# Retention and two gated MLPs on one core: first tile kept in SBUF, folding quarters and weight splits moved

## What is computed

```python
scores = (1 / sqrt(64)) * (q @ k.T)              # 8 batches x 8 heads, 576 x 576, head size 64
ret    = scores * gamma[h] ** (i - j), 0 for i < j
x      = ret @ v                                 # as 4608 tokens x 512
h      = max(max(x @ w1, x @ w2), x @ w3)        # 512 -> 768
x2     = h @ w_out                               # 768 -> 512
a, b   = x2 @ u1, x2 @ u2                        # 512 -> 1024
out    = ((a * b) @ u3) @ u_out                  # 1024 -> 1024 -> 512
```

## Time and profile before

| | us |
|---|---|
| three runs | 1256.33, 1257.79, 1263.64 |
| their median | 1257.79 |
| the profiled execution | 1263.11 |
| its span, first to last instruction | 1261.3 |
| TensorE busy in it | 1229.0 (97%) |
| VectorE, ScalarE, GpSimd busy | 774.1, 487.2, 434.0 |

### The profile page before, as it was taken

One profiled execution on the slowest core, in us unless ns is written; L12 is line 12 of the kernel. 1 busy time (PEld: TensorE's weight loads), 2 busy tenths in 40 slices (PEclk: granted clock), 3 DMA queues, 4 the chain that ended last, 5 costly groups with the idle time before them and its releaser, 6 DMA issues. The chain is left out here.

```text
span 1261.3 us, 21125 instructions
## 1 busy us (share of the span) xinstructions
PE 1229.0 (97%) x8288; PEld 1211.0 (96%) x8288; DVE 774.1 (61%) x1186; ACT 487.2 (39%) x771; POOL 434.0 (34%) x228
## 2 busy tenths in 40 slices
PE   7899999999999999999999999999999999999999
PEld 7798889999999999999999999999999999999998
DVE  5565676764645454558789767554545465867563
ACT  3333344432323242426455444242424243545441
POOL 2635536502020202033786564202020216266540
PEclk9899999999999999999999999999999999999999
DMA  9899865212020302033545441212121343444441
GB/s 328 313 333 349 297 235 160 86 47 79 26 101 26 100 26 95 32 126 126 192 163 198 163 169 57 102 64 106 50 101 57 107 156 123 151 150 151 156 157 64
DMA packets 87828, 174.15 MB, mean 138 GB/s; under 512 B 9648, under 2 KB 58416, under 8 KB 87728
## 3 DMA queue, kind: packets, MB, share of 16 engines
q1 hardware_dynamic: 79088, 163.94, 37.0%
q10 hardware_dynamic: 8640, 8.85, 2.0%
HBM read 109.32 MB, written 63.44 MB: 137 GB/s over the span
## 5 line engine op out<-in xcount | busy, mean ns | idle before, releaser
L1057 PE MATMUL ps<-chi,whi 128*128 128x384 f32 x2016 | 675.5, 335 | 11.6 <-DVE clo L795 5.9
L1059 PE MATMUL ps<-chi,wlo 128*128 128x384 f32 x2016 | 674.1, 334 | 0.0
L1058 PE MATMUL ps<-clo,whi 128*128 128x384 f32 x2016 | 674.1, 334 | 0.0
L554 POOL TENSOR_TENSOR raw<-raw,raw 128x768 f32<-128x768 f32 (+2 forms) x96 | 267.3, 2804 | 591.5 <-DMA raw<-xd 222.1
L1057 PEld LDWEIGHTS ps<-chi,whi 128*128 128x128 f32 x2016 | 378.9, 188 | 15.8 <-issue 7.9
L1058 PEld LDWEIGHTS ps<-clo,whi 128*128 128x128 f32 x2016 | 378.9, 188 | 0.0
L1059 PEld LDWEIGHTS ps<-chi,wlo 128*128 128x128 f32 x2016 | 378.9, 188 | 0.0
L795 DVE TENSOR_TENSOR clo<-raw,chi 128x768 fp32r<-128x768 f32 (+2 forms) x168 | 251.9, 1527 | 27.7 <-ACT chi L712 27.7
L712 ACT CAST chi<-raw 128x768 fp32r<-128x768 f32 (+2 forms) x168 | 180.3, 1080 | 86.0 <-PE ps L1059 52.3
L785 ACT COPY w<-ps 128x384 f32<-128x384 f32 x126 | 60.7, 482 | 253.4 <-PE ps L1059 252.0
L771 ACT COPY u<-ps 128x384 f32<-128x384 f32 x126 | 60.8, 482 | 161.8 <-PE ps L1059 160.1
(11 more groups left out here) (41 smaller groups left out, 857.0 us busy)
## 6 DMA issues: line engine op xcount, KB each, us to landing
qks<-qk SPq DMA_DIRECT2D x32, 576.0 KB, 7.0
gd<-h SPq DMA_DIRECT2D x96, 192.0 KB, 1.9
raw<-gd SPq DMA_DIRECT2D x24, 768.0 KB, 5.9
hd<-h SPq DMA_DIRECT2D x72, 192.0 KB, 1.9
raw<-hd SPq DMA_DIRECT2D x24, 576.0 KB, 5.6
vs<-vv SPq DMA_DIRECT2D x32, 320.0 KB, 8.4
raw<-xd SPq DMA_DIRECT2D x24, 384.0 KB, 5.7
x2d<-h SPq DMA_DIRECT2D x48, 192.0 KB, 2.1
```

Of the source, the lines that this page charges most:

```text
L554: return nc.gpsimd.tensor_tensor(out_, a, b, op)
L1057: nc.tensor.matmul(to, w1, x1, start=(start and k == 0), stop=False, skip_group_check=True)
L1058: nc.tensor.matmul(to, w1, x2, start=False, stop=False, skip_group_check=True)
L1059: last = nc.tensor.matmul(to, w2, x1, start=False, stop=(k == KH[st] - 1), skip_group_check=True)
```

## The change

- Outputs of the attention that belong to tile 0 (all of the first batch, the first 192 tokens of the second) are copied by ScalarE from PSUM into tile 0's raw blocks, and neither stored nor loaded. Later pairs go through three buffers `xst` in place of two, and SP issues their stores, behind v's loads.
- v is loaded as 512 columns and a tail of 64 rows; the zeros of the tail are set once by six memsets.
- The quarters are spread 0 in steps 0 to 3, 1 in steps 4 to 7, 2 in steps 8 to 11, 4 in steps 12 to 16. `uo` is loaded one piece per step in steps 2 to 5, `u3raw` in steps 1, 6, 8, 10 to 14, now behind the queries' load. GpSimd splits `uo` behind the queries.
- Weight blocks 9, 10, 19 and 20 are split one unit earlier, 20 is loaded one unit earlier, 11 to 13 are split at the end of the unit before (AT_ONCE), and the tokens of tile 0 of O are split at other points.

```diff
-HI_IO = {("prev", "w"): [0], ("end", "u"): [1], ("end", "p3"): [2], ("end", "p2"): [3],
+HI_IO = {("prev", "p3"): [0], ("end", "u"): [1], ("end", "p3"): [2], ("end", "p2"): [3],
...
-LO_IO = {("end", "21"): [0], ("end", "12"): [1], ("next", "22"): [2, 3], ("next", "12"): [4, 5, 6]}
+LO_IO = {("prev", "12"): [0], ("end", "12"): [1], ("next", "22"): [2, 3], ("next", "21"): [4],
+         ("next", "12"): [5, 6]}
...
-             18: 69, 19: 109, 20: 112}
+             18: 69, 19: 109, 20: 111}
...
-W_SPLIT_AT = {wi: it + (wi >= FIRST_W[C]) for wi, it in W_SUM_AT.items()}
+W_SPLIT_AT = {wi: it + (FIRST_W[I] <= wi < FIRST_W[O]) for wi, it in W_SUM_AT.items()}
+
+AT_ONCE = (11, 12, 13)
...
-WC_FROM = 3
-QUARTERS = 4 * FT2
+QUARTERS = [0] * 4 + [1] * 4 + [2] * 4 + [4] * 5
 
 
...
-    if m >= STEPS - 2:
-        return range(QUARTERS - 4 * (STEPS - m), QUARTERS - 4 * (STEPS - m) + 4)
-    return range(2 * (m - WC_FROM), 2 * (m - WC_FROM) + 2) if m >= WC_FROM else ()
...
-U3_LOAD = {min(2 * kb + WC_FROM - 2, STEPS - 3): kb for kb in range(FT2)}
-U3_SPLIT = {min(2 * kb + WC_FROM - 1, STEPS - 2): kb for kb in range(FT2)}
-UO_LOAD = {1: (0, 1), 2: (2, 3)}
-UO_SPLIT = {2: (0, 1), 3: (2, 3)}
-WC_READ = {min(2 * kb + WC_FROM + 1, STEPS - FT2 + kb): kb for kb in range(FT2)}
+    return range(sum(QUARTERS[:m]), sum(QUARTERS[:m + 1]))
+
+
+assert len(QUARTERS) == STEPS and sum(QUARTERS) == 4 * FT2
+
+U3_LOAD = {1: 0, 6: 1, 8: 2, 10: 3, 11: 4, 12: 5, 13: 6, 14: 7}
+U3_SPLIT = {3: 0, 7: 1, 9: 2, 11: 3, 12: 4, 13: 5, 14: 6, 15: 7}
+UO_LOAD = {2: 0, 3: 1, 4: 2, 5: 3}
+UO_SPLIT = {3: 0, 4: 1, 5: 2, 6: 3}
+WC_READ = {7: 0, 9: 1, 11: 2, 12: 3, 13: 4, 14: 5, 15: 6, 16: 7}
 P1_W_LOAD = {8: 0, 9: 1}
 P1_W_SUM = {9: (0, 0), 10: (0, 1), 11: (1, 0), 12: (1, 1)}
 P1_W_HI = {11: 0, 13: 1}
 P1_W_LO = {12: (0, 0), 13: (0, 1), 14: (1, 0), 15: (1, 1)}
-P1_RAW = 9
+
+TILE0 = [[(0, N, {0: 0, 1: 2}, 0), (N, SEQ, {0: 3, 1: 6}, 0)], [(0, 2 * N - SEQ, {0: 3, 1: 6}, SEQ - N)]]
+X_STORES = [0 if n < PAIRS else 1 if n < 2 * PAIRS else 2 for n in range(NP)]
+
+
+def x_stores(n):
+    return sum(X_STORES[i] for i in range(n % 3, n + 1, 3))
+
+
 P1_T = {10: 0, 11: 1, 12: 2, 13: 3}
 P1_HI = {12: 0, 13: 1, 14: 2, 15: 3}
 P1_LO = {13: 0, 14: 1, 15: 2, 16: 3}
 
 
-def build(nc, qk, vv, kk, wB, wC, wI, u3T, uo, decay, qdecay, vdecay, outT):
+def build(nc, qk, vv, vt, kk, wB, wC, wI, u3T, uo, decay, qdecay, vdecay, outT):
     f32, f32r = mybir.dt.float32, mybir.dt.float32r
     ALU = mybir.AluOpType
...
+        xst = at("xst", [P, 3, SEQ], f32, A21_AT + 3 * KH[B] * P * 4)
+        assert A21_AT + 3 * KH[B] * P * 4 + 3 * SEQ * 4 <= H_AT + 4 * N * 4
 
...
-                sp.dma_start(vs[n % 6][:, :], vv[n, :, :]).then_inc(v_loaded[n % 6], 16)
+                sp.dma_start(vs[n % 6][:, 0:NC * CH], vv[n, :, :]).then_inc(v_loaded[n % 6], 16)
+                sp.dma_start(vs[n % 6][TAIL:P, NC * CH:], vt[n, :, :]).then_inc(v_loaded[n % 6], 16)
 
...
                 half = 3 * b // 2
                 cut = N if b % 2 == 0 else SEQ - N
-                for i, (lo, hi) in enumerate(((0, cut), (cut, SEQ))):
-                    to = 0 if (b % 2 == 0 or i == 1) else N - cut
-                    sp.dma_start(acts[B][half + i, p // 2, :, p % 2, to:to + hi - lo], xst[:, n % 2, lo:hi]
-                                 ).then_inc(x_stored[n % 2], 16)
+                pieces = ((0, cut, 0 if b % 2 == 0 else N - cut), (cut, SEQ, 0))
+                for i, (lo, hi, to) in enumerate(pieces):
+                    if i >= 2 - X_STORES[n]:
+                        sp.dma_start(acts[B][half + i, p // 2, :, p % 2, to:to + hi - lo], xst[:, n % 3, lo:hi]
+                                     ).then_inc(x_stored[n % 3], 16)
 
             def load_u3(kb):
...
+                    load_weight(P1_W_LOAD[m])
+                for n in made_in(m + 2):
+                    load_qk(n)
                 if m in U3_LOAD:
                     load_u3(U3_LOAD[m])
-                for i in UO_LOAD.get(m, ()):
-                    load_uo(i)
-                if m in P1_W_LOAD:
-                    load_weight(P1_W_LOAD[m])
-                if m == P1_RAW:
-                    load_raw(0)
-                for n in made_in(m + 2):
-                    load_qk(n)
                 for n in (2 * m, 2 * m + 1):
                     if n + 4 < NP:
                         load_v(n + 4)
+                    if n - 2 >= PAIRS:
+                        store_x(n - 2)
                 if m in WC_READ:
                     store_wc(WC_READ[m])
-            for n in (NP - 2, NP - 1):
-                store_x(n)
 
...
             for m in range(STEPS - 1):
-                if m in U3_SPLIT:
+                if m in U3_SPLIT and m not in UO_SPLIT:
                     split_u3(U3_SPLIT[m])
-                for i in UO_SPLIT.get(m, ()):
-                    split_uo(i)
                 if m in P1_W_SUM:
                     sum_weight(*P1_W_SUM[m])
                 if m in P1_T:
                     combine(0, P1_T[m])
                 for n in made_in(m):
                     decay_queries(n)
+                if m in UO_SPLIT:
+                    if m in U3_SPLIT:
+                        split_u3(U3_SPLIT[m])
+                    split_uo(UO_SPLIT[m])
 
...
-                if n >= 2:
-                    act.wait_ge(x_stored[n % 2], 32 * (n // 2))
-                nc.scalar.copy(xst[:, n % 2, :],
-                               ps[:, 2 * (n % 2):2 * (n % 2) + 2, :].rearrange("p a b -> p (a b)")[:, 0:SEQ]
-                               ).then_inc(x_out, 1)
-
-            def store_x(n):
-                b, p = divmod(n, PAIRS)
-                act.wait_ge(x_out, n + 1)
-                half = 3 * b // 2
-                cut = N if b % 2 == 0 else SEQ - N
-                for i, (lo, hi) in enumerate(((0, cut), (cut, SEQ))):
-                    to = 0 if (b % 2 == 0 or i == 1) else N - cut
-                    act.dma_start(acts[B][half + i, p // 2, :, p % 2, to:to + hi - lo], xst[:, n % 2, lo:hi]
-                                 ).then_inc(x_stored[n % 2], 16)
+                x = ps[:, 2 * (n % 2):2 * (n % 2) + 2, :].rearrange("p a b -> p (a b)")
+                in_tile = TILE0[b] if b < 2 else []
+                for i, (lo, hi, block, to) in enumerate(in_tile):
+                    copy = nc.scalar.copy(raw[B][block[p // 2]][:, p % 2, to:to + hi - lo], x[:, lo:hi])
+                if X_STORES[n]:
+                    if n - 3 >= PAIRS:
+                        act.wait_ge(x_stored[n % 3], 16 * x_stores(n - 3))
+                    lo = in_tile[-1][1] if in_tile else 0
+                    copy = nc.scalar.copy(xst[:, n % 3, lo:SEQ], x[:, lo:SEQ])
+                copy.then_inc(x_out, 1)
 
             def split_uo(i):
...
                         split_weight(wi, 1)
+                for wi in AT_ONCE:
+                    if W_SPLIT_AT[wi] == it:
+                        split_weight(wi, 0)
+                        split_weight(wi, 1)
                 if it < G:
                     act.wait_ge(prod, DONE[(it, P7)])
...
             for i in range(2):
                 nc.vector.memset(state[i][:, :, :], 0.0).then_inc(zeroed, 1)
-            dve.wait_ge(zeroed, 6)
+            for i in range(6):
+                nc.vector.memset(vs[i][0:TAIL, NC * CH:], 0.0).then_inc(zeroed, 1)
+            dve.wait_ge(zeroed, 12)
             for m in range(STEPS):
```

More of the change, by code:

```diff
@@ L309, in build @@
         x_out = sem("x_out")
-        x_stored = [sem(f"x_stored{i}") for i in range(2)]
+        x_stored = [sem(f"x_stored{i}") for i in range(3)]
         uo_loaded = [sem(f"uo_loaded{i}") for i in range(4)]
@@ L431, in load_raw @@
                 if st == B:
-                    for i in range(2):
-                        sp.wait_ge(x_stored[i], 32 * (4 if t == 0 else NP // 2))
+                    for n in range(NP - 3, NP):
+                        sp.wait_ge(x_stored[n % 3], 16 * x_stores(n))
                 else:
@@ L438, in load_raw @@
                 if t == 0:
-                    if st != B:
-                        sp.wait_ge(c_lo, 7 * tau)
+                    sp.wait_ge(c_lo, 7 * tau)
                     if st == C:
@@ L581, in combine @@
                     for k in (0, 1):
-                        pool.wait_ge(raw_loaded[k], 16 * (tau + 1))
+                        pool.wait_ge(raw_loaded[k], 16 * tau)
+                    if tau == 0:
+                        pool.wait_ge(x_out, 2 * PAIRS)
                     if again:
@@ L588, in combine @@
                 if i == 1:
-                    pool.wait_ge(raw_loaded[2], 16 * (tau + 1))
+                    pool.wait_ge(raw_loaded[2], 16 * tau)
                     pool.wait_ge(combined, 4 * tau + 1)
@@ L598, in combine @@
                 if i == 3:
-                    pool.wait_ge(raw_loaded[3], 16 * (tau + 1))
+                    pool.wait_ge(raw_loaded[3], 16 * tau)
                     pool.wait_ge(combined, 4 * tau + 2)
@@ L644, in decay_values @@
```

(27 more changed lines are left out.)

5 lines of the change are left out of this document (4 added, 1 removed).

## The result

| | us |
|---|---|
| before, median of 4 runs | 1258.14 |
| changed, median of 4 runs | 1272.70 (1270.78 to 1275.85) |
| ratio, 95% interval | 1.0111 (1.0073 to 1.0148) |
| span of the profiled execution, before and changed | 1261.3, 1270.4 |
| first product of the later stages at | 193.04, 206.42 |

The change made the kernel 1.1% slower where 1.1% faster was forecast, and the time lies outside the range. The later stages take 4.3 us less. The first stage takes 13.4 us more. Step 8 starts at 81.22 and not at 91.53, so up to there the changed kernel is 10.3 us ahead; it loses 23.7 us behind that point.

What follows compares the result with a forecast made beforehand. Bound: TensorE, nearly always busy in 1068.3 us of later products, and a first stage losing 16.4 us to stalls. Span 1261.3 - 9.1 - 8.0 = 1244.2, plus 1.8 is 1246.0; less half of 5.3, 1243.5 us; range 1234 to 1254.

Steps and rivals of the forecast that it cites:

- What bounds the kernel now: First stage: TensorE's steps should take 153.3 us from step 2 but take 169.7, so 16.4 us are lost.
- First tile kept: First stage: dropping early stores and read back aims at 3.5 + some 2.8 us and slow clock (4.6 + 1.8).
- Quarters moved: First stage: the new spread sums to 155.6 us, 2.3 more than before, paying only through avoided stalls.
- Stalls that stay: Steps 3 to 11: transfers leave 0 to 9 us of stall, 5 taken; stage ends at 183.9, -9.1 us (-14 to -4).
- Stores on SP's queue: First stage: up to 16 issues per step on SP, costed at nothing beyond the 5 us of stall.
- Rival D: First stage: SP's issues become the bound, 13.3 us a step instead of 9.5, +34 us, 1278; chance 0.05.
- Later stages: Behind 193 us: earlier weight splits remove TensorE's waits, -8.0 us (-10.6 to -3), with new waits of 0.6 us three times.
- B: First stage: transfers bound it anyway at 318 GB/s, 9 us of stall stay, stage -0.5, 1252; chance 0.24.
- E: Later stages: the new split place costs as much as the old, -3 there, 1248.5; chance 0.12.
- a slower one: Whole kernel: a time above the 1% bound of 1270.4 us; chance 0.06.

Runs made afterwards that it cites:

- e8: e7 with the stores of the finished pairs issued by ScalarE and not SP; 1243.9 us, 0.9857 of the kernel before.
- e13: e8 with v loaded in one piece of 640 columns again, zeros included; 1244.5 us, 0.9884 of the kernel before.
- e12: e8 with two buffers for the finished pairs in place of three; 1248.4 us, 0.9925 of the kernel before.
- e6: e3 with the stores of the finished pairs issued by ScalarE, quarters spread as in the change; 1248.8 us, 0.9918 of the kernel before.
- e4: The kernel before with only the later stages' edits (weight and token splits moved, block 20 loaded earlier); 1257.5 us, 0.9968 of the kernel before.
- e14: e8 with weight block 9 of stage C split a unit later, where it was before the change; 1242.5 us, 0.9867 of the kernel before.
- e1: The changed kernel with SP issuing u3's load ahead of the step's weights and queries; 1251.5 us, 0.9941 of the kernel before.
- e7: e1 with quarters, uo and u3 loads and splits, and GpSimd's order as in the kernel before; 1250.0 us, 0.9907 of the kernel before.
- e3: The changed kernel with u3 loaded ahead of the queries and its low part behind the queries' decays on GpSimd; 1248.9 us, 0.9923 of the kernel before.
- e5: The changed kernel with the stores of the finished pairs issued by ScalarE, three buffers kept; 1267.7 us, 1.0055 of the kernel before.

## Why the prediction was wrong

**What bounds the kernel now**: right. The losses of the first stage were where it put them; with the tile kept and the ring loosened they go (e8: steps 4 to 12 all at 10.12 or 10.13 us).

**First tile kept**: right. With old quarters and ScalarE's stores the first product comes 12.5 us earlier (193.0 to 180.5). That the tile carries most of it is shown by exclusion only, since no run has the tile alone: with v whole the gain stays (e13), and with two buffers it stays in the trace's first stage (180.9), though the times are some 4 us longer (e12). One cost put at nothing was not nothing: in e8 TensorE waits 1.8 us at step 3 for the copies into the raw blocks, which ScalarE makes behind its rounding of `uo`.

**Quarters moved**: the sum was 2.3 us more for TensorE, and e6 against e8 gives 2.3 us. That it fits so well is partly luck, since two traces of one first stage differ by 0.9 us (before and e4, e8 and e14). Steps 4 and 5, with one quarter each, were priced at 8.9 us and take 9.6 and 9.7 in e1. With ScalarE's stores the spread buys nothing, since the stalls it was to avoid are gone without it. With the stores on SP's queue, as in the change, it seems to save some: e1's first product comes 3.4 us before e7's.

**Stalls that stay, 5 us (0 to 9)**: this is the step that failed. It priced the stage by bytes over a rate, and the change list has u3's load behind the queries' load, yet no term of the sum was made for that move. The queries' load waits for GpSimd, GpSimd for ScalarE, ScalarE for u3. The ring was in the code to be read, and in the trace of before GpSimd's decays stand behind the low part of u3:

```profile
97.90 2.36 POOL L554 TENSOR_TENSOR u3lo<-u3raw,u3hi 128x1024 fp32r<-128x1024 f32 x1 [7.61 <-ACT u3hi L683]
100.22 2.51 POOL L554 TENSOR_TENSOR qdec<-qks,qtab 128x512 f32<-128x512 f32 x2
```

On top of the 5 us the runs show 23.3 us for this move (first product at 206.4 against 183.1 in e1). Without it the forecast of that point, 183.9, was met within 1 us, and the stalls of e1 from step 2 on are 4.3 us (183.1 - 23.2 - 155.6). They are not all where they were put: 2.4 us lie in steps 4 to 7, whose price was low. By the prediction's own terms the stage's gain had to end at -5 and not at -4.

**Stores on SP's queue, nothing**: wrong with the old quarters, where they cost 6 us of the first stage (e7 against e8), right with the spread (e3 against e6). Rival D, SP issuing without a pause from step to step, is not what happened: its queue stood still for some 4.9 us before 83.79, waiting. From 83.79 to 94.95 it did issue without a pause, but e5, with fewer issues there, gained nothing at that place.

**Later stages, -8.0 (-10.6 to -3)**: right in sign, a mis-sized term; -4.3 in the trace, and -4.4 in e4. The new waits at the pairs of stage C were forecast well, 0.6 us three times: e8 has 0.8, 0.9 and 0.9, with pairs of 4.6 us where 2 to 4 were taken. But the list did not hold block 9, which the same table moves: its split met GpSimd at 560 and took 5.84 us, and TensorE waited 2.1 us for it (the kernel before has waits of 0.6 and 1.2 us at this stage change, at 599.76 and 604.34). Nor did it hold a wait of 1.5 us in stage O. There are these waits on VectorE's sums now:

```profile
PE ps L1075 <- DVE h L897: 5.6, 4, 2.2
PE ps L1075 <- DVE w L897: 1.5, 1, 1.5
```

(changed kernel, behind the first product), against 5.9 and 4.0 and 0.8 in the earlier trace rows. The waits for low halves are down to 0.4 us, as forecast.

**The rivals**: B asked for DMA engines that stay busy, and from 128.5 on they were busy 0.56 of the time. E, a split place as dear as the old one, came true at one of three places in e3, e6 and e13, where GpSimd started first. None of the rivals named the ring; the case that came was a slower one, which had 0.06.

## What to carry to other kernels

When a load moves down a queue, follow its waits round: what does it now stand behind, who releases that, and does that one wait for the load itself, a step earlier? Such a ring sets the step by the sum of its delays, however idle the DMA engines are, and here it was enough to give it one step more at one place. A store whose buffer is needed again can leave late in a queue of loads that wait; here that cost 6 us with the old quarters and nothing with the spread, so look whether a copy waits for it.

## What the runs showed of the hardware

A store did not land later for being on the queue of the loads: 5.6 us in the median on SP's, 5.9 on ScalarE's. What differs is when it is issued: 6.6 us behind its copy on SP's queue (e7: copy ended at 43.90, store at 50.53) and 0.3 us behind it on ScalarE's (e8: 44.69 and 44.99).

The granted clock of TensorE fell to 1.2 GHz (0.50 from 149 to 154) at its wait of 6.13 us in the changed kernel, is 0.93 in the mean of that kernel's last 78 us of the stage, and is 1.00 in the mean of e1's and e8's whole span, where only the wait at the kernel's start is longer than 2.2 us.

Two elementwise instructions of VectorE on weights (128x768 and 128x1024) took 4.56 us in e8 when they started 0.55 us ahead of GpSimd's run of differences, 6.98 us in e6 when GpSimd was 0.16 us ahead, and 2.08 us at another place of e6 (634.98), where GpSimd started 0.86 us behind them. So tenths of a microsecond decide between 2 and 7 us.
